# The first three experts of a routed mixture: rounding of w1, turning of tokens, and extra products put in another order

## The reference

```python
logits = x @ w_gate
order = np.argsort(-logits.flatten())
for idx in order:                      # best pairs (token, expert) first
    tok, e = (int(idx) // E, int(idx) % E)
    if assigned[tok] >= 0 or counts[e] >= cap:
        continue
    assigned[tok] = e
    counts[e] += 1
for e in range(E):
    mask = assigned == e
    h = np.maximum(x[mask] @ w1[e], 0.0)
    out[mask] = h @ w2[e]
```

## Time and profile before

| | |
|---|---|
| time, median of 3 runs | 1180.08 us (1179.22 to 1182.33) |
| the profiled execution | time 1181.97 us, span 1180.3 us |
| PE busy | 1085.2 us, 92% of the span |
| DVE, ACT, POOL busy | 639.8, 463.3, 416.7 us |
| mean granted clock of PE, 757.6 to 783.7 us | 0.50 |
| mean granted clock of PE, 60 to 756 us | 1.00 |
| 16 DMA engines, mean over the span | 85 GB/s |

### The profile page before, as it was taken

How to read it: one execution, slowest core, us unless ns; L and a number is a source line. 1 busy time by engine, 2 the same in 40 slices (tenths; PEclk the granted TensorE clock), 3 DMA queues, 4 the chain that set the end, 5 groups by cost and what they waited for, 6 DMA issues and landing times. The chain is left out here.

```text
span 1180.3 us, 21631 instructions
## 1 busy us (share of the span) xinstructions
PE 1085.2 (92%) x8225; PEld 907.4 (77%) x8225; DVE 639.8 (54%) x2204; ACT 463.3 (39%) x1167; POOL 416.7 (35%) x467
## 2 busy tenths in 40 slices
PE   2799999999999999999999999628898999999996
PEld 1488888888888888888888888527676777878995
DVE  4754656565656565656565645264545657663210
ACT  2665444444444444444444433112223233333441
POOL 1333222222222222222222223215357366566772
PEclk9999999999999999999999999857978999999998
DMA  6641312111111111111111000022405233423420
GB/s 192 209 134 51 139 53 69 50 67 52 66 54 67 51 69 51 66 54 68 52 66 51 28 10 19 19 94 78 169 29 178 91 123 129 170 73 142 180 98 27
DMA packets 19147, 100.02 MB, mean 85 GB/s; under 512 B 2800, under 2 KB 2800, under 8 KB 16848
## 3 DMA queue, kind: packets, MB, share of 16 engines
q0 software_dynamic: 9824, 58.99, 14.1%
q1 hardware_dynamic: 9216, 39.61, 10.0%
HBM read 86.00 MB, written 12.85 MB: 84 GB/s over the span
## 5 line engine op out<-in xcount | busy, mean ns | idle before, releaser
L321 POOL TENSOR_TENSOR g_low<-g,g_high 128x256 fp32r<-128x256 f32 x192 | 148.6, 774 | 503.5 <-ACT g_high L499 503.5
L417 PE MATMUL up_ps<-x_high,w_high 128*128 128x256 f32 x768 | 224.7, 293 | 0.0
L417 PE MATMUL up_ps<-x_low,w_high 128*128 128x256 f32 x768 | 214.9, 280 | 0.0
L417 PE MATMUL up_ps<-x_high,w_low 128*128 128x256 f32 x768 | 214.5, 279 | 0.0
L633 DVE SCALAR_TENSOR_TENSOR g<-g,up_ps 128x256 f32<-128x256 f32 x192 | 80.5, 419 | 226.1 <-ACT g L492 226.1
L417 PEld LDWEIGHTS up_ps<-x_high,w_high 128*128 128x128 f32 x768 | 145.0, 189 | 28.1 <-issue 22.1
L430 PE MATMUL down_ps<-w_high,g_low 128*128 128x512 f32 x384 | 152.1, 396 | 0.0
L430 PE MATMUL down_ps<-w_low,g_high 128*128 128x512 f32 x384 | 152.0, 396 | 0.0
L430 PE MATMUL down_ps<-w_high,g_high 128*128 128x512 f32 x384 | 151.7, 395 | 0.0
L622 DVE CUSTOM_DVE_ANT_0 product<-x,w_raw 128x512 f32<-128x512 f32 x176 | 147.2, 837 | 3.0
L417 PEld LDWEIGHTS up_ps<-x_low,w_high 128*128 128x128 f32 x768 | 145.0, 189 | 4.9
(11 more groups left out here) (183 smaller groups left out, 1940.8 us busy)
## 6 DMA issues: line engine op xcount, KB each, us to landing
qk_t<-qk_rows SPq DMA_DIRECT2D x24, 720.0 KB, 4.6
v_w<-v_win SPq DMA_DIRECT2D x24, 464.0 KB
w_raw<-weights SPq DMA_DIRECT2D x16, 512.0 KB, 5.2
x_rest<-x_any POOLq DMA_DIRECT2D x24, 256.0 KB, 4.6
x_rows<-x POOLq DMA_DIRECT2D x12, 512.0 KB, 3.2
w_raw<-gate_rows SPq DMA_DIRECT2D x1, 2048.0 KB, 9.5
x_g<-x_rows,token_index POOLq DMA_INDIRECT x24
out<-y,token_index POOLq DMA_INDIRECT x24
```

What stands on the lines that cost most here:

```text
L321: pool.tensor_tensor(g_low[:, u % 2, :], g[:, u % 2, :], g_high[:, u % 2, :].bitcast(F32), ALU.subtract)\
L417: last = nc.tensor.matmul(up_ps[:, u % 2, 0:GT * P], a[:, f, w], x[:, grp % 2, c, :], start=k == 0, stop=k == 3 * C - 1)
```

## The change

Five things are moved or added, all in `routed_experts`:

1. Experts 0 and 1 (those not turned early) turn their chunks into four banks: 0 and 1 into `up_ps` as before, 2 and 3 into `down_ps[0]` and `down_ps[1]` (`turned_at`). The wait of the chunks 2 and 3 is no longer for DVE, but (expert 1) for ACT's copies of expert 0's tiles 0 and 1.
2. For these two, the first up piece waits chunk by chunk for `x_low`, not for all four.
3. Expert 2 is turned behind m = 47 and m = 51 of expert 1, in the place of m = 39 and m = 47 (`turned_behind`); the experts 3 to 7 stay.
4. ACT: the eight roundings of expert 1's w1 stand ahead of `keep_y(0, 2)`; for p = 1 the roundings of w1 all stand ahead, then `keep_y(1, 0)`, half of the tokens, `keep_y(1, 1)`, the other half, `keep_y(1, 2)`.
5. `keep_busy`: in round 0, 10 products behind `sum_marks` and 12 behind `list_tokens`, of 192 columns in plain f32 (`logits` moving, `ident` as weights), into the bank `down_ps[2]`. Nothing reads them, and they wait for nothing.

```diff
-        TURN_BEHIND = (FC * C + FC - 1, FC * C + 2 * FC - 1)
-
         def turns_early(p):
             return 2 <= p < E
+
+        def turned_behind(p, m):
+            half = FC * C + FC
+            behind = (half + FC - 1, half + FC + FC // 2 - 1) if p == 1 else (half - 1, half + FC - 1)
+            return behind.index(m) if turns_early(p + 1) and m in behind else None
+
+        def turned_at(p, c):
+            if turns_early(p) or c < 2:
+                return up_ps[:, c % 2, 0:CAP]
+            return down_ps[:, c - 2, 0:CAP]
...
-                    if c >= 2:
+                    if c >= 2 and turns_early(p):
                         pe.wait_ge(x_low_ready, p * C + c - 1)
+                    elif c >= 2 and p:
+                        pe.wait_ge(y_ready, (p - 1) * CT + c - 1)
                     elif p:
                         pe.wait_ge(hidden_low_ready, p * FC)
                     for t in range(CT):
-                        last = nc.tensor.transpose(up_ps[:, c % 2, t * P:(t + 1) * P],
+                        last = nc.tensor.transpose(turned_at(p, c)[:, t * P:(t + 1) * P],
                                                    x_g[:, p % 2, t, c * P:(c + 1) * P], ident[:, :])
...
-                    if f == 0:
+                    if f == 0 and turns_early(p):
                         pe.wait_ge(x_low_ready, p * C + C)
...
+                        if f == 0 and not turns_early(p):
+                            pe.wait_ge(x_low_ready, p * C + c + 1)
...
                         if f < FC - 1:
-                            between(p * MM + FC * C + t * FC + f)
+                            between(p * MM + m)
+                            if turned_behind(p, m) is not None:
+                                turn_tokens(p + 1, turned_behind(p, m))
...
-                    if m in TURN_BEHIND and turns_early(p + 1):
-                        turn_tokens(p + 1, TURN_BEHIND.index(m))
+                    if turned_behind(p, m) is not None:
+                        turn_tokens(p + 1, turned_behind(p, m))
+
+            def keep_busy(count):
...
+                for _ in range(count):
+                    nc.tensor.matmul(down_ps[:, CT - 1, 0:T * E], ident[:, :], logits[:, :], start=True, stop=True)
...
                 route(0, k)
+                if k == SUMS:
+                    keep_busy(10)
+                if k == LIST:
+                    keep_busy(12)
...
                 for t in range(CT):
-                    if p + 1 < E and t < 2 and p:
+                    if p == 0 and t == 2:
+                        for f in range(FC):
+                            round_w1(p + 1, f)
+                    if 0 < p < E - 1 and t < 2:
                         for f in range(t * FC // 2, (t + 1) * FC // 2):
                             round_w1(p + 1, f)
-                    if t < 2 and turns_early(p + 1):
-                        round_tokens(p + 1, t)
-                    keep_y(p, t)
-                if p == 0:
-                    for f in range(FC):
-                        round_w1(p + 1, f)
+                    part = t - 1 if p == 1 else t
+                    if 0 <= part < 2 and turns_early(p + 1):
+                        if p == 1:
+                            keep_y(p, t - 1)
+                        round_tokens(p + 1, part)
+                    if p != 1 or t == CT - 1:
+                        keep_y(p, t)
```

More of the change, by code:

```diff
@@ L1487, in _ @@
                         decide(r, k)
[L1488 to L1489 removed]
+                    if turned_behind(p, m) is not None:
+                        rest_tokens(p + 1, turned_behind(p, m))
 def program(nc, qk_rows, v_win, q_t_heads, k_t_heads, v_rows, n_global, n_local, weights, gate, gate_rows, w1_rows, w2_rows, out,
```

7 lines of the change are left out of this document (3 added, 4 removed).

## The result

The changed kernel takes 1162.24 us (median of 4 runs, 1160.48 to 1165.71), the kernel before 1180.9 us in the same comparison (4 runs): ratio 0.985, interval 0.983 to 0.9869. It is faster by 18.7 us, and its time lies 1.2 us above the forecast range. The profiled execution took 1162.08 us, with a span of 1160.4 us, 19.9 less than that of the kernel before.

What follows compares the result with a forecast made beforehand. PE's own products bound the experts' steady part, with losses at the seams. Gains of 3.1 + 2.7 + 6.9 + 4.1 + 7.1 = 23.9 us led to a forecast of 1156.2 us, range 1153.5 to 1161.

Steps and rivals of the forecast that it cites:

- nothing waits for the clock on the wall and gives it back: Downstream, rounds 3 to 7 and POOL's gathers: paced by PE's steps in unchanged order, so no gain is lost again.
- term 4: Expert 1's up part: the clock stays at 1.00 instead of 0.50, so searches and products run faster; 4.1 us.
- term 5: Expert 2's tokens, turned behind another tile: the 4.5 us gap and the half clock behind it go; 7.1 us.
- term 2: Expert 0's start: unread products raise the clock and it holds, so about 18.5 products run at full clock; 2.7 us.
- first rival: Before expert 0 the clock falls in the gap from 795 to 799.6; 21 us off, 1159.0; chance 0.27.
- term 1: Expert 0's start: four banks and chunkwise waits bring the first up product earlier; 3.1 us, 2.7 at half clock.
- term 3: Expert 1's start: w1 rounded ahead, tokens turned without waiting, first up product at 853.0 instead of 859.90; 6.9 us.
- the signs given for a wrong prediction: `list_ps` later than 790.4, ACT waiting for `w_raw` at 845, or `eup_ps` waiting for `ex_low` at expert 2's beginning.
- what the profile was to show: Clock 1.00 from about 787 to 790 and at 800, earlier first up products, no half clock in expert 1.

Runs made afterwards that it cites:

- the later two: Two more profiles of the changed kernel, unedited; the kernel timed 1163.62 and 1164.59 us in those comparisons.
- parts_banks_w1: Kernel before with only the four banks, the chunkwise wait and expert 1's w1 rounded ahead: 1172.16 us, ratio 0.9938.
- after_again: Changed kernel run once more with no edit, against the kernel before: 1163.62 us, ratio 0.9856.
- held_no_scatter: Changed kernel with 20 unread products for 12, w2's first rounding behind the Relu, unread products at three lists, no scatters for experts 0 and 1: 1158.21 us.
- after_fill20: Changed kernel with 20 unread products in place of 12 behind round 0's list_tokens: 1165.22 us, ratio 0.9883.

## Why the prediction was wrong

The direction was right, and the time came at the places that were forecast; the sum was 5 to 8 us too large, and the range ended 1.2 us too low. The step that failed is "nothing waits for the clock on the wall and gives it back", with the full clock that the terms 4 and 5 took for granted: short waits that the kernel had or that the moves brought to light were put at nothing. (That term 2 could lose its clock was the first rival.) In the first profile the lost clock and the late signals cost 1.3 us in the terms 1 and 2, 1.2 in term 5 and 1.35 behind expert 2; in the later two, where a signal of PE comes late in term 4 as well, 1.9 to 2.5 us more there.

- **Term 1**, 3.1 us. Measured 2.7 for the first up product (9.53 us behind list 0, 12.25 before; 2.9 and 2.2 in the later profiles), the value that was given for half clock. Right in size.
- **Term 2**, 2.7 us. Mis-sized: 1.8, from the 4.5 us that both terms gave, and with the wrong cause. The clock fell at 799.0, among the transposes behind the 2.87 us wait for the tokens, and the first six up products ran at 0.50. So the first rival occurred in part, with a stretch of 3.4 us and not of six. Without any unread product the first count is only 0.25 to 0.3 us later, and the clock is back as soon: what came beyond term 1 came with the earlier start. With 20 products in place of 12 the missing 1.2 us came, in this segment.
- **Term 3**, 6.9 us. Measured 6.8 (6.4 and 6.7 in the later profiles). Right, and shown by parts_banks_w1; alone the banks bring 2.6 of it and the early rounding 4.7.
- **Term 4**, 4.1 us. Measured 4.4 in the first profile, 1.6 and 2.2 in the later ones. What failed here is that three rounds of search need 2.94 us each at full clock, as in expert 0 (8.8 us): it is 8.65 us in the first profile (849.57 to 858.22) and 10.22 in after_again (849.43 to 859.65). Expert 0's search runs while POOL issues nothing (none between 798 and 831 us); expert 1's runs while it issues expert 0's scatters. One signal is 1.5 us late and a digit waits 1.3 us for it, and a half-clock stretch behind it takes the rest. That the first profile shows the forecast's size is luck: its count was answered 0.05 us ahead of the issue. The trace of the kernel before has a weak sign of it:

```profile
865.24 0.97 POOL L1099 DMA_INDIRECT out<-y,token_index  x1 [0.30 <-issue]
865.31 0.80 PE L1128 MATMUL search_ps<-wants,cmp 128*31 128x8 bf16 x24
865.94 0.56 DVE L1472 SCALAR_TENSOR_TENSOR hidden_low<-eup_ps,hidden_high 128x384 fp32r<-128x384 f32 x1 [1.36 <-ACT hidden_high L1274]
866.83 0.15 DVE L1344 CUSTOM_DVE_ANT_0 enough<-search_ps,places 31x8 f32<-31x8 f32 x1 [0.33 <-PE search_ps L1128]
```

DVE answered this count 1.52 us behind its start, where the counts around it (861.16, 869.48) were answered in 0.84. Half of the difference is `hidden_low`, which DVE did first; 0.33 us are left in which it waited for a count whose record had ended. At half clock no digit waited for it.
- **Term 5**, 7.1 us. Measured 5.9 in all three. The wait for tokens and its slow products went as forecast (held_no_scatter: 7.2 us). 1.2 to 1.3 us were lost again, as a half-clock stretch in one profile and as a late hand-over in the others.
- **"Nothing ... gives it back."** This sentence failed: from expert 2 to the end 1.35 to 1.5 us are lost to one half-clock stretch behind round 4's list. The kernel before had the same wait there of 1.54 us, and no such stretch in its one profile.
- The sum was made from one profile, and from its terms at their full size. Nothing in it was left for stretches at half clock behind short waits, though the waits at the lists (1.41, 1.54 and 1.20 us) were in the trace.

Of the signs given for a wrong prediction one came, by 0.3 us (`list_ps` at 790.70); ACT did not wait at 841 to 845, and there was no wait at expert 2's beginning. Of what the profile was to show, two things did not come: the clock at 800 is 0.50, the sign of the first rival, and expert 1 has a stretch at 0.50 (880.9 to 884.3).

Shown: the share of the scatters in terms 4 and 5 (without them and at full clock the ledger's sum is 24.1 us off, where 23.9 were forecast, though by a kernel with 8 more unread products, unread products at the lists and w2 rounded later), the fall of the clock before expert 0, the two edits behind term 3. Open: what makes PE's signals late while POOL issues an indirect DMA, and whether PE's work stands still then; and why the clock falls behind one short wait in one execution and not in the next. The same kernel's profiles show both, so one profile cannot say which edit removed such a stretch.

## What to carry to other kernels

Price a removed wait net of what comes back with it. At each seam ask which other engine's issues now fall into the uncovered work, and leave room for the short waits that remain ahead of dense products. Waits of 1.0 to 1.5 us were followed by a stretch at half clock in some executions here and not in others; a stretch of 3.4 us cost 1.4 to 1.6 us, the ones of 10 and 14 us in expert 0 cost 4.6 and 4.7. Filling a wait with unread products moved the changed kernel's first count by 0.3 us where they ended 2.9 us ahead of the transposes, and by 1.5 us where they reached up to them; neither shows in the medians. Before you call two edits more than their sum, look at the intervals: 1.9 and 4.2 us alone and 8.3 together are within them. Where effects are 1 to 2 us, profile the same kernel several times: its own profiles differed by 3 us in the routed stage, and the profiled execution can be the fastest of its kernel.

## What the runs showed of the hardware

- In dense down products the granted clock fell to 0.50 for 3.4 us, 2.0 us behind the end of a wait of 1.42 us (878.86 to 880.9), and rose again; eight products cost 1.6 us more.
- Twelve transposes directly behind dense products left the clock at 1.00 (0.87 and 0.82 us for six in after_fill20, against 1.54 at half clock in the earlier trace rows).
- A plain f32 product of 192 columns shows as two records and takes 0.32 to 0.35 us at full clock, 0.64 at half (784.29 to 784.93 in the changed kernel), against 0.17 at full clock for a product of 384 columns of rounded operands.
- Around POOL's issues of indirect DMAs (0.94 to 1.01 us each) PE's signals came up to 2.1 us late, to DVE and to ACT: 138 of the 805 signals near such an issue were more than 0.15 us late, none of the 3681 others, and none of another engine. **The Trainium skill**, "SBUF — State Buffer", section "SBUF: two separate sides", names a pair of ports that VectorE and GpSimd hold in turn, for VectorE operations in a two-port mode or with two inputs in SBUF. The VectorE operation that starts late here reads one operand from PSUM, and ScalarE is late as well, so that rule does not cover this case.
